# A second router kept as rows of eight, and eleven filler products ahead of a sort, in a fused recurrence and two mixtures of experts

## The reference, cut to what matters

```python
for t in range(S):                       # B, H, S, D = 4, 8, 768, 40
    y[:, :, t] = einsum('bhd,bhde->bhe', rt, state)
    Sa = einsum('bhde,bhe->bhd', state, at)
    state = state * wt - outer(Sa, bt) + outer(vt, kt)
x = attn_out.transpose(0, 2, 1, 3).reshape(3072, 320)

def layer(x):                            # twice, with other weights
    logits = x @ w_gate                  # 320 -> 8
    e = argmax(logits); gate = softmax(logits)[e]   # first layer: times a sigmoid
    h = maximum(x[mask_e] @ w1[e], 0)    # 320 -> 1024
    out[mask_e] = gate * (h @ w2[e])     # 1024 -> 320
```

## Time and profile before

| | us |
|---|---|
| median of 3 runs | 1289.96 (1289.43 to 1297.5) |
| profiled execution, own time | 1287.04 |
| its span, first to last instruction | 1285.3 |
| PE busy | 1097.9 (85%) |
| DVE busy | 558.7 (43%) |
| ACT busy | 396.4 (31%) |
| POOL busy | 302.4 (24%) |

### The profile page before, as it was taken

One profiled execution on the slowest core, in us unless ns is written; L12 is line 12 of the kernel. 1 busy time (PEld: TensorE's weight loads), 2 busy tenths in 40 slices (PEclk: granted clock), 3 DMA queues, 4 the chain that ended last, 5 costly groups with the idle time before them and its releaser, 6 DMA issues.

```text
span 1285.3 us, 41335 instructions
## 1 busy us (share of the span) xinstructions
PE 1097.9 (85%) x18328; PEld 949.7 (74%) x18328; DVE 558.7 (43%) x864; ACT 396.4 (31%) x550; POOL 302.4 (24%) x253
## 2 busy tenths in 40 slices
PE   1189894888898889986899999999569999997997
PEld 0188784777888878885788888888448888876885
DVE  6635363364536443416176777767650111110111
ACT  0033332333333334331333333333004333323330
POOL 5440443043034213000112122121201212121111
PEclk8557997896888689777799999999868999998999
DMA  3333439343334333216024224333300331443000
GB/s 84 93 96 84 101 88 68 78 95 81 95 74 110 81 88 74 56 40 199 18 74 146 66 77 129 98 115 103 87 7 29 123 107 61 141 139 112 21 11 1
DMA packets 143115, 107.64 MB, mean 84 GB/s; under 512 B 91553, under 2 KB 120233, under 8 KB 142813
## 3 DMA queue, kind: packets, MB, share of 16 engines
q1 hardware_dynamic: 130560, 84.99, 25.0%
q0 software_dynamic: 6016, 16.05, 3.9%
q10 hardware_dynamic: 6364, 3.96, 2.0%
HBM read 87.51 MB, written 22.09 MB: 85 GB/s over the span
## 4 chain that ended last, share of the span: by engine, by line
PE 76%; DVE 8%; issue 7%; POOL 3%; DMA 3%; ACT 2%; SPq 1%; ACTq 0%; POOLq 0%; DVEq 0%
PE pair L1179 19%; PE pair L1160 17%; PE pair L1167 5%; PE pair L986 4%; PE bank L1054 3%; PE pair L1147 2%; PE pair L875 2%; PE pair L1073 2%; POOL AG L575 2%; PE bank L969 2%; PE bank L1062 2%; PE pair L892 2%; PE pair L924 2%; PE bank L1136 2%; PE pair L909 2%
## 5 line engine op out<-in xcount | busy, mean ns | idle before, releaser
L1179 PE MATMUL pair<-abk_own,H_nat 128*128 x992 | 277.7, 433 | 1.7 <-DVE S_nat L1451 1.7
L1160 PEld LDWEIGHTS pair<-H_nat,rvm 128*128 128x128 f32 x1984 | 238.3, 197 | 23.0 <-ACT H_nat L665 14.2
L1160 PE MATMUL pair<-H_nat,rvm 128*128 128x128 f32 x1984 | 239.6, 281 | 11.9 <-ACT H_nat L665 11.9
L1179 PEld LDWEIGHTS pair<-abk_own,H_nat 128*128 128x128 f32 x992 | 183.9, 190 | 71.3 <-issue 2.7
L665 ACT ACTIVATE rvm<-ring_own 128x2560 f32 x62 | 145.0, 2339 | 149.5 <-issue 86.0
L816 ACT ACTIVATE H_nat<-pair 128x512 f32<-128x512 f32 x62 | 37.0, 596 | 289.4 <-PE pair L1167 289.4
L1451 DVE TENSOR_SCALAR S_nat<-pair,gate_all 128x320 f32<-128x320 f32 x62 | 34.1, 551 | 206.1 <-PE pair L1179 206.1
L1444 DVE TENSOR_SCALAR H_nat<-pair 128x512 f32<-128x512 f32 x62 | 42.5, 686 | 167.0 <-PE pair L1167 167.0
L575 POOL TENSOR_TENSOR AG<-abk_own,F_run 40x512 f32<-40x512 f32 x48 | 60.3, 1257 | 173.9 <-DVE T_nat L1254 143.5
L589 POOL TENSOR_SCALAR_AFFINE_SELECT AG<-AG 64x512 f32<-64x512 f32 x48 | 43.1, 899 | 202.6 <-ACT AG L665 200.2
L646 POOL DMA_INDIRECT between<-S_nat,token_all x31 | 33.9, 1094 | 234.7 <-DVE S_nat L1462 226.6
(11 more groups left out here) (137 smaller groups left out, 1501.2 us busy)
## 6 DMA issues: line engine op xcount, KB each, us to landing
abk_own<-w SPq DMA_DIRECT2D x16, 1280.0 KB, 8.6
ring_own<-w SPq DMA_DIRECT2D x16, 512.0 KB, 3.6
ring_own<-w SPq DMA_DIRECT2D x32, 256.0 KB, 4.6
t_dram<-T_rows SPq DMA_DIRECT2D x12, 384.0 KB, 2.4
ring_own<-w SPq DMA_DIRECT2D x32, 128.0 KB, 5.2
w_in<-wT SPq DMA_DIRECT2D x48, 80.0 KB
abk_own<-aT SPq DMA_DIRECT2D x24, 160.0 KB
abk_own<-bT SPq DMA_DIRECT2D x24, 160.0 KB
```

The lines of the kernel that those rows point to most:

```text
L1160: mm(to, w1_now[:, par, k * F + m * P:k * F + m * P + P], xT[:, (0, 2 - m // 4)[k], :], start=(m % 4 == 0 and k == 0), stop=False, skip_gr ...
L1179: last = mm(bank[5][:, 0:DM], hidT[par][:, k, :], ring2[:, bass.ds(place, 1), k, :].rearrange("p a d -> p (a d)"), start=(k == 0), stop=(k ...
```

## The change

Three things change.

1. `wr_dram` is 320 rows of 8, as in `router_w`. The copy into it moves whole rows of 8 numbers (32 bytes) in place of 2560 single ones, and DVE reads `wr_next` with a step of 8 elements instead of one after the other. `turn_router` is renamed.
2. `WARM` is 11 in place of 6, in both layers.
3. `lg_parts` has two places in place of 24; ACT waits, before it writes one, until DVE has summed what was there two sets before.

```diff
-WARM = 6
+WARM = 11
...
-        lg_parts = sb("lg_parts", [P, NG, NPAIR, 2 * E])
+        lg_parts = sb("lg_parts", [P, 2, 2, NPAIR, 2 * E])
...
-        terms, wr_next = [part(AG[:, :, :, :, :, :].rearrange("p u o b a t -> p (u o b a t)"), n * E * DM, E, DM)
-                          for n in range(2)]
+        A_flat = AG[:, :, :, :, :, :].rearrange("p u o b a t -> p (u o b a t)")
+        terms = part(A_flat, 0, E, DM)
+        wr_next = part(A_flat, E * DM, DM, E)
...
-        wr_dram = nc.dram_tensor("wr_dram", [E, DM], F32, kind="Internal").ap()
+        wr_dram = nc.dram_tensor("wr_dram", [DM, E], F32, kind="Internal").ap()
...
-            sp.dma_start(wr_next, wr_dram.unsqueeze(0).to_broadcast([P, E, DM])).then_inc(wr_landed, 16)
+            sp.dma_start(wr_next, wr_dram.unsqueeze(0).to_broadcast([P, DM, E])).then_inc(wr_landed, 16)
...
-                copy(lg_parts[:, 2 * s * NT + t:(2 * s + 1) * NT + t + 1:NT],
+                if k >= 2:
+                    act.wait_ge(lg_summed, k - 1)
+                copy(lg_parts[:, k % 2],
...
-            def turn_router():
-                act.dma_start(wr_dram, router_w[1, :, 0:E].rearrange("d e -> e d"),
-                              allow_slow_non_contiguous=True).then_inc(wr_turned, 16)
+            def load_next_router():
+                act.dma_start(wr_dram, router_w[1, :, 0:E]).then_inc(wr_turned, 16)
...
-                v.tensor_reduce(lg_all[:, here, :], lg_parts[:, here].rearrange("p g a x -> p g x a"),
+                v.tensor_reduce(lg_all[:, here, :], lg_parts[:, k % 2].rearrange("p g a x -> p g x a"),
...
-                    v.tensor_tensor(terms, wr_next[:, :, :],
+                    v.tensor_tensor(terms, wr_next.rearrange("p d e -> p e d"),
```

More of the change, by code:

```diff
@@ L796, in _ @@
                     if c == 1 and j == 2:
-                        turn_router()
+                        load_next_router()
             for s in range(2):
```

## The result

The changed kernel takes a median of 1352.11 us (1347.11 to 1363.87, 4 runs) against 1289.7 (1288.81 to 1297.5) for the kernel before, measured beside it. The ratio is 1.048, with a 95% interval of 1.040 to 1.057. The range of the prediction, 1262 to 1284, is missed by far, and on the wrong side.

What follows compares the result with a forecast made beforehand. It took a 16.2 us overlong recurrence slot, PE's slow clock in the sorts, and PE, then DVE at the end, in the first layer as bounds. -15.2 - 8.8 + 4.0 = -20.0 from 1289.96 gave 1270.0, range 1262 to 1284.

Steps and rivals of the forecast that it cites:

- The copy as rows: Recurrence, slot after the copy into `wr_dram`: 320 pieces instead of 2560 gain 15.2 us, bounds 10.3 and 20.3.
- the 1.0 that I kept for the 320 pieces: Recurrence, same slot: 1.0 us of stall assumed to remain with 320 pieces, taken between nothing and 2.1.
- PE's stalls are late instructions: Recurrence, slot after the copy: PE's 17.1 us of stalls inferred to be instructions not fetched in time by crowded transfer engines.
- The fillers: Both sorts: more filler products keep PE at 2.4 GHz for the 48-record list, 4.4 us each, 8.8 together.
- lg_parts: Recurrence: ACT's wait for a DVE sum two slots ahead costs zero.
- The read's own price: First layer's DVE multiply L1458: reading with a step of 8 adds 2.0 us, 2825 ns becoming 4.86 us.
- The 4.0 at the end of the layer: First layer's last two tiles: the longer multiplies stand in the chain and cost 4.0 us, bounds 0.3 and 7.0.
- In a tile's steady state 2.0 hides in the 2.59 that DVE stands: First layer's tiles: the 2.0 us longer multiply fits in DVE's 2.59 us idle before `result`, 0.6 left, no cost.
- The slow one: First layer's tiles: rival where the stepped read costs 3.5 us per multiply and DVE becomes the bound, 1299 us; chance 0.08.
- slower by over 1%: Whole kernel: a time above 1302.9 us, given a chance of 0.06.
- The rival in which the copy crowds as before: Recurrence: 320 pieces hold up instruction fetch as long as 2560, the slot stays long, 1285 us; chance 0.07.
- that in which the clock falls: Both sorts: PE's clock falls ahead of the list or rises too late, fillers only delay it, 1281 us; chance 0.09.

Runs made afterwards that it cites:

- rows only: The dense version with six filler products in place of eleven, so the copy by rows without the fillers: 1271.44 us against 1286.61 for the kernel before, ratio 0.990.
- both: The dense version with POOL's gathers also issued one tile earlier: 1263.81 us against 1285.75 for the kernel before, ratio 0.983.
- gather: The changed kernel, stepped read kept, with each POOL gather issued one tile earlier, ahead of the send: 1257.1 us, ratio 0.983 to the kernel before.
- dense version: The changed kernel, but DVE copies the second router once into a dense tile that every multiply reads: 1257.88 us against 1282.08 before, ratio 0.982.
- the sum before the multiply: The dense version plus an unread DVE sum of 1800 elements in each first-layer tile, placed before the multiply: 1306.14 us, one execution.
- the same sum after it: The dense version plus the same unread sum of 1800 elements, placed after each first-layer tile's multiply: 1324.37 us, one execution.

## Why the prediction was wrong, point by point

- **The copy as rows: right.** Forecast 15.2. The slot gave 19.1, the recurrence 24.3 in the profiled pair, and 15.8 between the means of six profiled kernels with rows (575.5, all but `rows only` and `both`) and of the three with the whole copy in single elements (591.3). The run without the fillers gave 12 us, with an interval of 7 to 18. No run can tell the 1.0 that I kept for the 320 pieces from nothing. That PE's stalls are late instructions stays an inference: no run tells it from another cause on the same transfer engines.
- **The fillers: right in their stage.** Forecast 8.8, measured 9.1 in the two sorts, with each list at 5.47 for 5.4. By themselves they made no difference to the time that the runs could show.
- **`lg_parts`: nothing forecast, and nothing seen.** No run tests it by itself.
- **The read's own price: right.** Forecast 2.0 us per multiply from one row of 192 elements, measured 4.820 less 2.825. DVE's idle before `result` was forecast at 0.6 and is 0.58 in the tiles that don't wait. The 4.0 at the end of the layer came out smaller: with the stepped read and no waits (`gather`) the tiles are 2.0 us longer than in the dense version and the way to the second routing 0.9, together 2.9.
- **"In a tile's steady state 2.0 hides in the 2.59 that DVE stands": this step failed, and with it the whole.** I asked whether DVE had room and whether `relu1` was in time, and named `send` as 2.0 later without asking who stands behind it. Behind the `send` of a tile POOL's list has the gather of the tile four further on, and PE turns those tokens before its next `down`. Two things were used up. The first is a place in a row: the gather had started 1.06 us ahead of each load of weights, and 2 us later it starts behind it and lands up to 7.5 us after its start, so the lateness alone cost 34 us (the sum before the multiply). The second is a gap: the gather had run for 1.02 us just ahead of the next multiply, and 2 us later it starts within it. That costs 20 us more with a multiply of 2.83 us (the same sum after it), and with one of 4.82 it brings the tiles to 92.
- **The row that would have told it was in the trace of the kernel before.** In the layer's last tiles the order of events is another one, and there one `send` falls under a multiply (920.88 to 923.70). The timeline of POOL:

```profile
921.15 3.41 POOL L646 DMA_INDIRECT between<-S_nat,token_all  x1 [8.13 <-DVE S_nat L1451]
```

  3.41 us, where all the other sends take 1.0, and its end at 924.56 is 0.86 after the multiply's. I read the chain of waits over that very place for the price of the multiply, and not POOL's row beside it.
- **The rivals.** The slow one was right that the read would turn the sign, and wrong in mechanism and size: DVE's own list (8.9 us) was never the bound. I gave slower by over 1% a chance of 0.06. The rival in which the copy crowds as before and that in which the clock falls did not come.

The Trainium skill ("SBUF — State Buffer", in the section "Who interferes with whom") says that a DVE instruction with two inputs in SBUF contends with a GpSimd instruction that reads SBUF, and one with a single input outside the 2-port modes does not. The orders of sum and multiply above fit it: 3.44 us beside the multiply, 1.02 beside the sum. But the multiply also writes 2560 elements of each partition where the sum writes one, and no run tells the two inputs from that. The same section of the Trainium skill says of descriptor generation that `tensor_tensor` was not seen to stall it. Here a `tensor_tensor` does hold up the instruction with which POOL issues a gather, 14 times of 27; these transfers take a list of tokens from the local memory, so a read may be in it, but no run here isolates that read.

## What to carry to other kernels

When an edit makes an instruction longer, follow not only its engine's room but every queue behind what it releases, to the next thing that engine issues, and ask what that will now run beside. Look in the trace for any instance of an instruction that took several times its usual length and see what ran beside it: one outlier among thirty is the price list of an overlap that the edit may make the rule. And a transfer issued on GpSimd that does not depend on the send ahead of it belongs ahead of that send.

## What the runs showed of the hardware that I had not expected

- A gather or scatter issued by POOL takes 1.02 us by itself, 3.44 us when it starts some 0.3 us after a DVE multiply of 2.83 us with both inputs in the local memory, and 5.30 us beside one of 4.82 us. It ends some 0.85 us after the multiply. Beside a DVE sum of 2.03 us with one input it takes 1.02 us, and also when it starts 0.75 us ahead of the multiply.
- Reading every eighth float32 costs a multiply of 2560 elements 2.0 us more (2.825 to 4.82), but a plain copy of the same 2560 elements with the same step took 2.51 us, less than even the dense multiply.
- Copying single float32 elements in DRAM costs far more than their bytes: beside 2560 of them (10 KB) a transfer of `t_dram` took 21.4 us to land in place of 2.4, and one slot was 19 us longer; 1280 made theirs some 14 us longer, and 320 rows of 32 bytes left no trace.
- The same gather landed 2.9 to 3.5 us after its start when it started 1.06 us ahead of a load of weights, and 5.1 to 7.5 us after it when it started up to 1.0 us behind.
